# A fused retention, routed-experts and gated-unit kernel on one core: low halves of streamed pieces moved from GpSimd to VectorE, one visit for the one-hot matrix

## The chip, the cores and the metric

The kernel runs on one core of a Trainium2 chip. The metric is the device time of one execution in microseconds (us).

## The reference

Three layers follow one another on N = 3072 tokens of width 512.

```
state = gamma*state + k_t v_t ;  y_t = scale * q_t state        # retention: 4 batches, 8 heads, 768 steps
logits = x @ w_gate                                              # [3072, 8]
order = argsort(-logits.flatten())                               # greedy: best (token, expert) pairs first,
  a token is given once, an expert takes at most cap = 384 tokens
out[mask_e] = relu(x[mask_e] @ w1[e]) @ w2[e]                    # w1 512x1024, w2 1024x512
gate = sigmoid(x @ Wg);  val = x @ Wv                            # Wg, Wv 512x1536
result = (gate * val) @ w_out                                    # 1536x512
```

## The kernel before, in words

**First stage (lines 262 to 638).** Retention over 24 units of 128 tokens. It writes the rows of x to memory and the router's logits to on-chip memory. GpSimd splits the first 16 resident weight pieces there.

**Second stage (lines 640 to 1226).** Eight rounds, one for each expert in the order in which experts fill. Every float32 operand is split into a high half (ScalarE copies it into a fp32r tile) and a low half (raw minus high), and each product is three matmuls: high by high, high by low, low by high (`three`, L1114; L1116 to L1118, and L1194 to L1196 for the output products). A round on TensorE, written out by hand in `one_round` (L1120), is:

- `h_tile(g)`, g = 0..7: 4 steps each, a step being 3 matmuls of 384 columns;
- `h2_tile(m)`, m = 0..3: 8 steps each;
- `gate_val(f)`, f = 0..11: 4 steps for the gate, 4 for the value, and after each but the first `out_products(f-1)`: 3 steps of 3 matmuls of 512 columns;
- four times three transposes of the next expert's gathered rows (L1111), and the last `out_products(11)`.

**Streamed pieces.** Of weights, 24 pieces of 128x512 go through an 8-deep ring in each round: 8 of w1, 8 of w2, 8 of w_out. SP loads one when its slot is free, ScalarE makes its high half (`piece_high`, L760), GpSimd its low half (`piece_low`, L711, an operation of L714), each in the order of the pieces. Only the first eight low halves of round 0 are made by VectorE (`first_low`, L997). Twelve resident pieces come late: ScalarE splits off their high halves before round 0 and GpSimd their low halves in round 0, two behind each streamed piece from number 16 on (`late_low`, L707, an operation of L259). They are first needed in `gate_val(8)`.

**Routing.** While round i runs, VectorE and TensorE find expert i+1 and its 384 tokens together. TensorE makes "visits": small matmuls between two steps, at places fixed by `visit_at` (L101), counted in matmul columns at 2200 to the planned microsecond. TensorE waits at a visit, in order, until VectorE's part (`route(vis)`, L876) is ready. There are 7 digits of 3 visits. The first visit of a digit (L1075) needs the comparison `above` (L852), which VectorE makes from `prefix` (L892) after the digit before. Then come a tie visit, a count visit, a rank visit (V_RANK, number 23, L1097), and four visits (L1102) with 6 one-hot matrices each, held in two buffers of six. After the last one VectorE computes the row numbers and prepares the next routing (`route_ids`, `close`, `prepare`, L960, L952, L856), as one unbroken run of small operations, and GpSimd gathers the rows (`gather`, L699).

**VectorE's order.** `one_round` (L1007) writes it out: before each main operation, `route_until(at)` puts in the routing parts whose planned time has come. The main operations are `h_low(g)`, `h2_low(m)`, and for every f `product(f)` (pf, L991, needs the value part of f) and, after ScalarE's ph (L784), `p_low(f)` (pl, L995), which `out_products(f)` needs. Planned times from the code: `h_end` runs 2.1 to 16.8, `h2_end` 20.9 to 33.5, `val_end[f]` = 37.7, 41.9, 48.2, 54.5, 60.7, 67.0, 73.3, 79.6, 85.9 and so on; `out_end[f-1]` is 2.1 after `val_end[f]`.

```
DIGIT_GAP, LATE_GAP, PART_GAP = us(6.8), us(5), us(4)
while vis[0] < VISITS and (vis[0] == 0 or visit_at[vis[0] - 1 - (vis[0] > V_IDS)] <= at): route(...)
if vis[0] == VISITS and visit_at[VISITS - 1] <= at: route_ids(i + 1); close(); prepare()
```

Of the kernel before, what the change touches and what calls it, by code (L numbers as in the profile page):

```python
# [16 lines left out]
def retention_moe_glu_kernel(nc, q, k, v, w_router, w1, w2, w_gate, w_val, w_out, decay, out):  # L17
# [14 lines left out]
    with ctx:  # L32
# [3 lines left out]
        def sem(name):  # L36
            return ctx.enter_context(nc.semaphore(name))
# [39 lines left out]
        PARTS = U // TPART  # L77
        VISITS = V_IDS + PARTS

# [17 lines left out]
        def us(t):  # L97
            return int(t * COLUMNS_PER_US)

        DIGIT_GAP, LATE_GAP, PART_GAP = us(6.8), us(5), us(4)  # L100
        visit_at = [us(1) + vis // 3 * DIGIT_GAP + us((0, 1.7, 4)[vis % 3]) for vis in range(3 * DIGITS)]  # L101
        visit_at += [visit_at[-1] + (n + 1) * LATE_GAP for n in range(4)]
        visit_at += [visit_at[-1] + (n + 1) * PART_GAP for n in range(PARTS - 1)]
        expert_at = visit_at[V_RANK]
        ids_at = visit_at[-1] + us(2)
        SPLIT_AFTER = us(5)
# [64 lines left out]
        at_above = nc.sbuf_base  # L171
        onehot = sb("onehot", [P, 2, TPART, P], BF16)

# [20 lines left out]
        ring_raw = [placed(f"ring_raw{n}", [P, 512], F32, at_ring + (2 * n + 1) * 512 * 4) for n in range(RING)]  # L194
        above = placed("above", [P, U, RADIX], BF16, at_above)
        digit_i = placed("digit_i", [P, DIGITS, U], I32, at_above)
# [3 lines left out]
        gate = placed("gate", [P, 2, CAP], F32, at_hh + 6 * CAP * 4)  # L200
        xg = placed("xg", [P, TT, DM], F32, at_hl)
        orow = placed("orow", [P, TT, DM], F32, at_h2l)
        shared = at_big + (RESIDENT - 3) * 2 * 512 * 4
# [7 lines left out]
        half_compared = sem("half_compared")  # L211
        route_done = sem("route_done")
        dve_chain = sem("dve_chain")
        expert_known = sem("expert_known")
# [482 lines left out]
        @block.gpsimd  # L697
        def _(pool):
            def gather(i):  # L699

                pool.wait_ge(ids_ready, i + 1)
                pool.sem_inc(ids_seen, 1)
                for j in range(TT):
                    pool.indirect_dma_start(out=xg[:, j, :], out_offset=None, in_=xrows[:, :],
                                            in_offset=bass.IndirectOffsetOnAxis(ap=ids[:, j:j + 1], axis=0)).then_inc(x_gathered, 16)

            def late_low(k):  # L707
                pool.wait_ge(resident_hi, EARLY + k + 1)
                resident_low(EARLY + k)

            def piece_low(i, n):  # L711
                s = n % RING
                pool.wait_ge(piece_hi, STREAMED * i + n + 1)
                nc.gpsimd.tensor_tensor(ring[:, s, 1, :], ring_raw[s][:, :], ring[:, s, 0, :].bitcast(F32),  # L714
                                        ALU.subtract).then_inc(piece_lo, 1)

            def scatter(i):
                pool.wait_ge(ids_kept, i + 1)
                nc.gpsimd.tensor_copy(out_ids[:, :], ids_all[:, bass.ds(i, 1), :].rearrange("p o j -> p (o j)")).then_inc(out_ids_ready, 1)
                pool.wait_ge(out_ids_ready, i + 1)  # L720
                for j in range(TT):
                    pool.wait_ge(orow_ready, TT * (i + 1) + j + 1)
                    pool.sem_inc(orow_seen, 1)
                    pool.indirect_dma_start(out=out[:, :], out_offset=bass.IndirectOffsetOnAxis(ap=out_ids[:, j:j + 1], axis=0),  # L724
                                            in_=orow[:, j, :], in_offset=None).then_inc(scattered, 16)
                pool.wait_ge(scattered, 16 * TT * (i + 1))
                pool.sem_inc(orow_free, 1)

            def one_round(i, follows, late):
                gathered = not follows  # L730
                for n in range(RING, STREAMED + RING if follows else STREAMED):
                    if not gathered and split_at[n] > ids_at:
                        pool.wait_ge(h_done, EVACUATED * (i + 1))
                        gather(i + 1)
                        gathered = True
                    piece_low(i, n)
                    if n >= 2 * RING:
                        for k in late[:2]:
                            late_low(k)
                        late = late[2:]  # L740
                if not gathered:
                    pool.wait_ge(h_done, EVACUATED * (i + 1))
                    gather(i + 1)
                scatter(i)

            gather(0)
            pool.wait_ge(piece_lo, RING)
            one_round(0, True, list(range(LATE)))
            with pool.Fori(1, E - 1) as i:
                one_round(i, True, [])  # L750
            one_round(E - 1, False, [])

# [69 lines left out]
        def _(dve):  # L822
# [53 lines left out]
            def route(vis, i):  # L876
# [3 lines left out]

                dve.wait_ge(route_done, i * VISITS + vis - (vis > V_IDS))
                if vis < V_TIE and vis % 3 == 1:
# [53 lines left out]
                elif vis == V_IDS:  # L936
# [7 lines left out]
                    link(nc.vector.scalar_tensor_tensor(row[:, :], thirds[:, :], -float(P), PS_K[:, 0:U], ALU.mult, ALU.add))  # L944
                if vis >= V_IDS:
                    n = vis - V_IDS
                    for t in range(TPART):
                        tile = n * TPART + t
                        last = nc.vector.tensor_scalar(onehot[:, n % 2, t, :], column[:, :], row[:, tile:tile + 1], None, ALU.is_equal)
                    last.then_inc(route_ready, 1)  # L950

# [44 lines left out]

            def first_low(n):  # L997
                dve.wait_ge(piece_hi, n + 1)
                nc.vector.tensor_tensor(ring[:, n, 1, :], ring_raw[n][:, :], ring[:, n, 0, :].bitcast(F32),
                                        ALU.subtract).then_inc(piece_lo, 1)  # L1000
# [6 lines left out]
            def one_round(i, follows):  # L1007
                vis = [0 if follows else VISITS + 1]

                def route_until(at):  # L1010

                    while vis[0] < VISITS and (vis[0] == 0 or visit_at[vis[0] - 1 - (vis[0] > V_IDS)] <= at):
                        route(vis[0], i + 1)
                        vis[0] += 1
                    if vis[0] == VISITS and visit_at[VISITS - 1] <= at:
                        route_ids(i + 1)
                        close()
                        prepare()
                        vis[0] += 1
# [3 lines left out]
                for g in range(KF):  # L1023
                    route_until(h_end[g] + us(0.3))
                    h_low(i, g)
                for m in range(KD):
                    route_until(h2_end[m] + us(0.3))
                    h2_low(i, m)
                for f in range(KG):
                    route_until(val_end[f])  # L1030
                    product(i, f)
                    route_until(val_end[f] + us(0.4))
                    p_low(i, f)
                assert vis[0] == VISITS + 1
                if follows:
# [11 lines left out]
            for vis in range(VISITS):  # L1047
                route(vis, 0)
            route_ids(0)
            close()  # L1050
            prepare()
            assert link_count[0] == ROUTE_CHAIN, link_count[0]
            for n in range(RING // 2):
                first_low(n)
            for a in range(KD):
                x_low(0, a)
            for n in range(RING // 2, RING):
                first_low(n)
            with dve.Fori(0, E - 1) as i:
# [4 lines left out]
        def _(pe):  # L1064
            pe.wait_ge(tables_made, TABLES)

            def visit(vis, i):
                if vis < V_TIE and vis % 3 == 0:

                    for t in range(0, U, FOLD):  # L1070
                        if t == 0:
                            pe.wait_ge(half_compared, i * DIGITS + vis // 3 + 1)
                        if t == U // 2:
                            pe.wait_ge(route_ready, i * VISITS + vis + 1)
                        last = nc.tensor.matmul(PS_R[:, 0:FOLD * E], above[:, t:t + FOLD, :].rearrange("p t r -> p (t r)"),  # L1075
                                                choice[:, :, t:t + FOLD], start=t == 0, stop=t == U - FOLD)
                    last.then_inc(route_done, 1)
                    return
                pe.wait_ge(route_ready, i * VISITS + vis + 1)
                if vis < V_TIE and vis % 3 == 1:  # L1080
# [18 lines left out]
                else:  # L1099
                    n = vis - V_IDS  # L1100
                    for t in range(TPART):
                        last = nc.tensor.matmul(PS_R[:, 0:2 * TT], onehot[:, n % 2, t, :],  # L1102
                                                slot_ids[:, n * TPART + t, :, :].rearrange("p j n -> p (j n)"),
                                                start=n == 0 and t == 0, stop=n == PARTS - 1 and t == TPART - 1)
                last.then_inc(route_done, 1)
# [156 lines left out]
```

## Time and profile before

| | |
|---|---|
| median of 3 runs | 1146.23 us (1145.22 to 1147.03) |
| the profiled execution | 1147.63 us, its span 1145.9 us |
| TensorE busy with matmuls | 1074.8 us of the span (94%) |
| VectorE busy | 563.3 us (49%) |
| ScalarE busy | 340.0 us (30%) |
| GpSimd busy | 368.0 us (32%) |
| mean granted TensorE clock | 0.971 of 2.4 GHz |

A profile is one execution. "Busy" counts the time in which an engine has an instruction in work. A wait is time in which an engine had none, and is put down to what ended it. Matmuls overlap one another, so that a matmul of 334 ns may be followed by the next after 174 ns.

### The profile page before, as it was taken

The page shows a single profiled execution, that of the slowest core. Times are in us where ns is not written, and L with a number is a line of the kernel's source. Part 1 is how long each engine was busy: PE and PEld are TensorE (multiplying, and loading weights), DVE is VectorE, ACT ScalarE, POOL GpSimd, SP SyncE. Part 2 cuts the span into 40 slices and gives each one's busy share as a digit, 9 for nine tenths or more (in the row PEclk, how much of TensorE's full clock was granted, in tenths as well). Part 3 has the DMA queues.
Part 4 walks back from the last instruction along what each step waited for, and adds up shares of the span by engine and source line. Part 5 has one row for each costly group of instructions (what it writes and reads, how often), then busy time and mean ns, then how long its engine had stood idle before and what let it go on. Part 6 is the DMA issues. An engine that isn't in the chain of part 4 may idle for free.

```text
span 1145.9 us, 20263 instructions
## 1 busy us (share of the span) xinstructions
PE 1074.8 (94%) x7544; PEld 989.7 (86%) x7544; DVE 563.3 (49%) x1431; ACT 340.0 (30%) x635; POOL 368.0 (32%) x357
## 2 busy tenths in 40 slices
PE   5999932989999999999999999999999999999996
PEld 5999922978999889998999899989998999899995
DVE  3555458565445554565356535563456356631111
ACT  2433322322233123412341234222322232224211
POOL 5443401480325042503250416041513151325101
PEclk9999965989999999999999999999999999999998
DMA  9999443311222122312231213121303140304000
GB/s 203 239 225 222 126 129 101 93 56 42 61 83 93 37 65 74 102 38 65 65 111 33 68 56 113 31 69 55 111 23 88 38 126 21 92 19 147 19 1 28
DMA packets 172960, 96.47 MB, mean 84 GB/s; under 512 B 80224, under 2 KB 158048, under 8 KB 172896
## 3 DMA queue, kind: packets, MB, share of 16 engines
q1 hardware_dynamic: 169056, 82.92, 27.1%
q0 software_dynamic: 3840, 12.59, 3.5%
q8 instruction: 53, 0.87, 0.3%
q14 instruction: 11, 0.09, 0.0%
HBM read 82.90 MB, written 12.58 MB: 83 GB/s over the span
## 4 chain that ended last, share of the span: by engine, by line
PE 75%; DVE 8%; issue 2%; POOL 0%; ACT 0%; DMA 0%; DVEq 0%; POOLq 0%
PE bank L1116 19%; PE bank L1118 18%; PE bank L1117 18%; PE bank L1194 6%; PE bank L1195 5%; PE bank L1196 5%; DVE above L852 2%; PE bank L1111 1%; DVE prefix L892 1%; PE bank L1075 1%; PE bank L1083 1%; DVE best L858 0%; DVE top L866 0%; PE bank L1102 0%; ACT ph L784 0%
## 5 line engine op out<-in xcount | busy, mean ns | idle before, releaser
L714 POOL TENSOR_TENSOR ring<-ring_raw,ring 128x512 fp32r<-128x512 f32 x184 | 238.3, 1300 | 435.6 <-ACT ring L764 420.9
L1116 PE MATMUL bank<-h2h,resident 128*128 128x384 f32 x768 | 263.8, 343 | 0.6 <-DVE h2l L982 0.2
L1118 PE MATMUL bank<-h2h,resident 128*128 128x384 f32 x768 | 258.6, 337 | 0.0
L1117 PE MATMUL bank<-h2l,resident 128*128 128x384 f32 x768 | 258.2, 336 | 0.0
L1116 PEld LDWEIGHTS bank<-h2h,resident 128*128 128x128 f32 x768 | 144.8, 189 | 4.5 <-DVE h2l L982 1.1
L1117 PEld LDWEIGHTS bank<-h2l,resident 128*128 128x128 f32 x768 | 144.8, 189 | 3.1
L1118 PEld LDWEIGHTS bank<-h2h,resident 128*128 128x128 f32 x768 | 144.6, 188 | 0.0
L764 ACT ACTIVATE ring<-ring_raw 128x512 fp32r<-128x512 f32 x192 | 117.5, 623 | 64.7 <-DMA ring_raw<-in_moe_w_out_dram 40.7
L991 DVE TENSOR_TENSOR pf<-bank,gate 128x384 f32<-128x384 f32 x96 | 53.1, 553 | 169.9 <-PE bank L1118 166.2
L784 ACT ACTIVATE ph<-pf 128x384 fp32r<-128x384 f32 x96 | 50.4, 525 | 245.5 <-DVE pf L991 245.5
L780 ACT ACTIVATE gate<-bank 128x384 f32<-128x384 f32 x96 | 47.1, 491 | 214.2 <-PE bank L1118 214.2
L1116 PE MATMUL bank<-xh,ring 128*128 128x384 f32 x256 | 90.9, 355 | 0.0
L1116 PE MATMUL bank<-hh,ring 128*128 128x384 f32 x256 | 90.6, 354 | 0.0
L1118 PE MATMUL bank<-xh,ring 128*128 128x384 f32 x256 | 86.5, 338 | 0.0
L1117 PE MATMUL bank<-xl,ring 128*128 128x384 f32 x256 | 86.4, 337 | 0.0
L1118 PE MATMUL bank<-hh,ring 128*128 128x384 f32 x256 | 85.9, 336 | 0.0
L1117 PE MATMUL bank<-hl,ring 128*128 128x384 f32 x256 | 85.8, 335 | 0.0
L724 POOL DMA_INDIRECT out_dram<-orow,out_ids x24 | 23.7, 986 | 183.0 <-DVE orow L1005 178.2
L1194 PE MATMUL bank<-ring,ph 128*128 128x512 f32 x192 | 78.5, 409 | 3.9 <-DVE pl L995 3.9
L995 DVE TENSOR_TENSOR pl<-pf,ph 128x384 fp32r<-128x384 f32 x96 | 54.4, 567 | 52.6 <-ACT ph L784 52.6
L1195 PE MATMUL bank<-ring,ph 128*128 128x512 f32 x192 | 76.2, 397 | 0.0
L1196 PE MATMUL bank<-ring,pl 128*128 128x512 f32 x192 | 76.1, 397 | 0.0
(168 smaller groups left out, 1745.1 us busy)
## 6 DMA issues: line engine op xcount, KB each, us to landing
ring_raw<-in_moe_w_dram SPq DMA_DIRECT2D x128, 256.0 KB, 3.0
ring_raw<-in_moe_w_out_dram SPq DMA_DIRECT2D x64, 256.0 KB, 2.9
qraw<-in_q_dram SPq DMA_DIRECT2D x24, 256.0 KB, 4.0
kraw<-in_k_dram SPq DMA_DIRECT2D x24, 256.0 KB, 4.8
vraw<-in_v_dram SPq DMA_DIRECT2D x24, 256.0 KB, 5.0
xrows<-xrow SPq DMA_DIRECT2D x24, 256.0 KB, 2.9
resident_raw<-in_moe_w_gate_dram SPq DMA_DIRECT2D x12, 256.0 KB, 4.6
resident_raw<-in_moe_w_val_dram SPq DMA_DIRECT2D x12, 256.0 KB, 4.7
```

Source lines behind the costliest of these rows:

```text
L714: nc.gpsimd.tensor_tensor(ring[:, s, 1, :], ring_raw[s][:, :], ring[:, s, 0, :].bitcast(F32), ALU.subtract).then_inc(piece_lo, 1)
L764: nc.scalar.activation(ring[:, n % RING, 0, :], ring_raw[n % RING][:, :], ACT.Copy).then_inc(piece_hi, 1)
L780: nc.scalar.activation(gate[:, f % 2, :], bank[2 * (f % 2)][:, 0:CAP], ACT.Sigmoid).then_inc(gate_ready, 1)
L784: nc.scalar.activation(ph[:, f % 2, :], pf[:, f % 2, :], ACT.Copy).then_inc(ph_ready, 1)
L991: nc.vector.tensor_tensor(pf[:, f % 2, :], bank[2 * (f % 2) + 1][:, 0:CAP], gate[:, f % 2, :], ALU.mult).then_inc(p_ready, 1)
L995: nc.vector.tensor_tensor(pl[:, f % 2, :], pf[:, f % 2, :], ph[:, f % 2, :].bitcast(F32), ALU.subtract).then_inc(pl_ready, 1)
L1116: nc.tensor.matmul(ps, wh, xhi, start=start, stop=False)
L1117: nc.tensor.matmul(ps, wh, xlo, start=False, stop=False)
L1118: return nc.tensor.matmul(ps, wl, xhi, start=False, stop=stop)
L1194: nc.tensor.matmul(PS_OUT[j][:, :], ph[:, f % 2, toks], wh, start=f == 0, stop=False)
L1195: nc.tensor.matmul(PS_OUT[j][:, :], ph[:, f % 2, toks], wl, start=False, stop=False)
L1196: last = nc.tensor.matmul(PS_OUT[j][:, :], pl[:, f % 2, toks], wh, start=False, stop=f == KG - 1)
```

## The change

VectorE makes all the low halves of streamed pieces, put into its written order by `splits_until`. GpSimd no longer makes them; its late resident ones are made one at a time in round 0, each after a gate or a value part of `gate_val(0)` to `gate_val(5)`. The 24 one-hot matrices get a buffer of their own, in the half of `hl` that the gathered rows leave free; VectorE makes them in four parts right behind one another without waiting for TensorE, and TensorE uses them in one visit. `above` no longer shares the one-hot buffers' memory.

```diff
-        VISITS = V_IDS + PARTS
+        VISITS = V_IDS + 1
-        DIGIT_GAP, LATE_GAP, PART_GAP = us(6.8), us(5), us(4)
+        DIGIT_GAP, LATE_GAP, PART_GAP = us(6.8), us(5), us(2)
-        visit_at += [visit_at[-1] + (n + 1) * LATE_GAP for n in range(4)]
-        visit_at += [visit_at[-1] + (n + 1) * PART_GAP for n in range(PARTS - 1)]
+        visit_at += [visit_at[-1] + (n + 1) * LATE_GAP for n in range(3)]
         expert_at = visit_at[V_RANK]
+        part_at = [expert_at + us(1) + n * PART_GAP for n in range(PARTS)]
+        visit_at += [part_at[-1] + LATE_GAP]
         ids_at = visit_at[-1] + us(2)
-        onehot = sb("onehot", [P, 2, TPART, P], BF16)
+        above = sb("above", [P, U, RADIX], BF16)
-        above = placed("above", [P, U, RADIX], BF16, at_above)
+        onehot = placed("onehot", [P, U, P], BF16, at_hl + TT * DM * 4)
...
 # gpsimd
-            def one_round(i, follows, late):
-                gathered = not follows
-                for n in range(RING, STREAMED + RING if follows else STREAMED):
-                    if not gathered and split_at[n] > ids_at:
-                        pool.wait_ge(h_done, EVACUATED * (i + 1))
-                        gather(i + 1)
-                        gathered = True
-                    piece_low(i, n)
-                    if n >= 2 * RING:
-                        for k in late[:2]:
-                            late_low(k)
-                        late = late[2:]
-                if not gathered:
+            def one_round(i, follows):
+                if follows:
                     pool.wait_ge(h_done, EVACUATED * (i + 1))
                     gather(i + 1)
                 scatter(i)
             gather(0)
-            pool.wait_ge(piece_lo, RING)
-            one_round(0, True, list(range(LATE)))
+            for k in range(LATE):
+                pool.wait_ge(val_done if k % 2 else gate_done, k // 2 + 1)
+                late_low(k)
...
 # vector
-                if vis >= V_IDS:
-                    n = vis - V_IDS
-                    for t in range(TPART):
-                        tile = n * TPART + t
-                        last = nc.vector.tensor_scalar(onehot[:, n % 2, t, :], column[:, :], row[:, tile:tile + 1], None, ALU.is_equal)
-                    last.then_inc(route_ready, 1)
+            def make_onehot(n, i):
+                if n == 0 and not (isinstance(i, int) and i == 0):
+                    dve.wait_ge(h_done, EVACUATED * i)
+                for tile in range(n * TPART, (n + 1) * TPART):
+                    last = nc.vector.tensor_scalar(onehot[:, tile, :], column[:, :], row[:, tile:tile + 1], None, ALU.is_equal)
+                last.then_inc(onehot_ready, 1)
-            def first_low(n):
+            def piece_low(i, n):
...
+                def splits_until(at):
+                    while split[0] < (STREAMED + RING if follows else STREAMED) and split_at[split[0]] + us(1.2) <= at:
+                        piece_low(i, split[0])
+                        split[0] += 1
                 def route_until(at):
-                    while vis[0] < VISITS and (vis[0] == 0 or visit_at[vis[0] - 1 - (vis[0] > V_IDS)] <= at):
+                    while vis[0] < VISITS and (vis[0] == 0 or visit_at[vis[0] - 1] <= at):
                         route(vis[0], i + 1)
                         vis[0] += 1
+                    while vis[0] == VISITS and part[0] < PARTS and part_at[part[0]] <= at:
+                        make_onehot(part[0], i + 1)
+                        part[0] += 1
...
                     h_low(i, g)
+                    splits_until(h_end[g])
...
                     h2_low(i, m)
+                    splits_until(h2_end[m])
...
                     p_low(i, f)
+                    splits_until(val_end[f] + us(2))
...
 # tensor
-                    n = vis - V_IDS
-                    for t in range(TPART):
-                        last = nc.tensor.matmul(PS_R[:, 0:2 * TT], onehot[:, n % 2, t, :], ...
+                    for t in range(U):
+                        if t % TPART == 0:
+                            pe.wait_ge(onehot_ready, i * PARTS + t // TPART + 1)
+                        last = nc.tensor.matmul(PS_R[:, 0:2 * TT], onehot[:, t, :], ...
```

## Rows read from the trace of the kernel before

**Rows 1.** The page's first part: busy time and share of the span, by engine.

```profile
PE 1074.8 (94%) x7544; PEld 989.7 (86%) x7544; DVE 563.3 (49%) x1431; ACT 340.0 (30%) x635; POOL 368.0 (32%) x357
```

**Rows 2.** Waits from 200 us on: engine, line, waited for; total us, times, longest.

```profile
PE bank L1075 <- DVE above L852: 5.3, 5, 1.3
PE bank L1194 <- DVE pl L995: 3.9, 7, 0.6
```

**Rows 3.** The chain that ended last: transposes that open rounds 0, 1 and 2; start, length.

```profile
196.97 2.82 PE bank L1111 x12
...
323.64 1.31 PE bank L1111 x12
...
440.40 1.31 PE bank L1111 x12
```

**Rows 4.** Stretches of round 0: length, busy by engine, granted clock, DMA share, GB/s.

```profile
230.00:240.00 10.00, 8.70 (x59) 8.11 (x58) 6.56 (x9) 3.13 (x6) 10.00 (x8) 1.00 0.28 100
240.00:250.00 10.00, 8.16 (x44) 7.18 (x44) 5.13 (x8) 3.60 (x7) 10.00 (x9) 0.83 0.18 54
250.00:260.00 10.00, 7.57 (x41) 6.25 (x40) 6.05 (x9) 0.91 (x2) 4.13 (x3) 0.83 0.00 0
```

**Rows 5.** TensorE in order of time, round 0: start, length, instruction, idle before it.

```profile
233.19 0.24 PE L1075 MATMUL bank<-choice,above 128*128 128x32 bf16 x3 [1.30 <-DVE above L852]
...
242.53 0.24 PE L1075 MATMUL bank<-choice,above 128*128 128x32 bf16 x3 [1.30 <-DVE above L852]
...
253.07 0.24 PE L1075 MATMUL bank<-choice,above 128*128 128x32 bf16 x3 [1.13 <-DVE above L852]
254.61 0.26 PE L1075 MATMUL bank<-choice,above 128*128 128x32 bf16 x3 [1.29 <-DVE above L852]
```

**Rows 6.** VectorE (round 0, then round 1) and GpSimd (round 0) in order of time.

```profile
238.00 1.31 DVE L892 SCALAR_TENSOR_TENSOR prefix<-prefix,bank,digit_f 128x24 f32<-128x24 f32 x1 [1.85 <-PE bank L1087]
239.35 3.13 DVE L852 TENSOR_TENSOR above<-prefix,ladder 128x384 bf16<-128x384 f32 x2
...
332.79 0.25 DVE L892 SCALAR_TENSOR_TENSOR prefix<-digit_f,bank 128x24 f32<-128x24 f32 x1
333.07 1.02 DVE L852 TENSOR_TENSOR above<-prefix,ladder 128x384 bf16<-128x384 f32 x2
...
240.48 3.13 POOL L259 TENSOR_TENSOR resident<-resident_raw,resident 128x512 fp32r<-128x512 f32 x2
```

**Rows 7.** Groups by line: low halves on GpSimd, then those on VectorE (ns: least, median, most).

```profile
L714 POOL TENSOR_TENSOR ring<-ring_raw,ring 128x512 fp32r<-128x512 f32 x184 | 238.3, 1300 | 435.6 <-ACT ring L764 420.9
...
L999 DVE TENSOR_TENSOR ring<-ring_raw,ring x8: 681/682/683, 195.3 to 202.6; 128x512 fp32r<-128x512 f32 x8
```

**Rows 8.** The last visit of round 1 and what follows it, TensorE and VectorE.

```profile
410.45 0.31 PE L1102 MATMUL bank<-slot_ids,onehot 128*128 128x6 bf16 x6
...
410.80 0.16 DVE L963 TENSOR_REDUCE id_sums<-bank 128x3 f32<-128x6 f32 x1 [3.21 <-PE bank L1102]
...
417.44 0.55 DVE L991 TENSOR_TENSOR pf<-bank,gate 128x384 f32<-128x384 f32 x1
418.58 0.56 DVE L995 TENSOR_TENSOR pl<-pf,ph 128x384 fp32r<-128x384 f32 x1 [0.59 <-ACT ph L784]
...
419.29 0.47 PE L1194 MATMUL bank<-ring,ph 128*128 128x512 f32 x1 [0.57 <-DVE pl L995]
```

**Rows 9.** Two steps of `gate_val` on TensorE, first matmul of each.

```profile
416.48 0.33 PE L1116 MATMUL bank<-h2h,resident 128*128 128x384 f32 x1
...
417.00 0.33 PE L1116 MATMUL bank<-h2h,resident 128*128 128x384 f32 x1
```

**Rows 10.** Round 1 around digit visit 18: VectorE, then TensorE.

```profile
369.51 0.56 DVE L995 TENSOR_TENSOR pl<-pf,ph 128x384 fp32r<-128x384 f32 x1 [0.59 <-ACT ph L784]
369.99 0.24 DVE L892 SCALAR_TENSOR_TENSOR prefix<-prefix,bank,digit_f 128x24 f32<-128x24 f32 x1
...
372.47 0.32 PE L1075 MATMUL bank<-choice,above 128*128 128x32 bf16 x6
```

More of the change, by code:

```diff
@@ L201, in retention_moe_glu_kernel @@
         xg = placed("xg", [P, TT, DM], F32, at_hl)
+        onehot = placed("onehot", [P, U, P], BF16, at_hl + TT * DM * 4)
+        assert TT * DM * 4 + U * P * 2 <= KF * CAP * 4
         orow = placed("orow", [P, TT, DM], F32, at_h2l)
@@ L212, in retention_moe_glu_kernel @@
         route_done = sem("route_done")
+        onehot_ready = sem("onehot_ready")
         dve_chain = sem("dve_chain")
@@ L709, in late_low @@
                 resident_low(EARLY + k)
[L711 to L715, printed above, removed]
             def scatter(i):
@@ L746, in _ @@
             gather(0)
-            pool.wait_ge(piece_lo, RING)
-            one_round(0, True, list(range(LATE)))
-            with pool.Fori(1, E - 1) as i:
-                one_round(i, True, [])
-            one_round(E - 1, False, [])
+            for k in range(LATE):
+                pool.wait_ge(val_done if k % 2 else gate_done, k // 2 + 1)
+                late_low(k)
+            with pool.Fori(0, E - 1) as i:
+                one_round(i, True)
+            one_round(E - 1, False)
         @block.scalar
@@ L879, in route @@
                     return
-                dve.wait_ge(route_done, i * VISITS + vis - (vis > V_IDS))
+                dve.wait_ge(route_done, i * VISITS + vis)
                 if vis < V_TIE and vis % 3 == 1:
@@ L995, in p_low @@
                 nc.vector.tensor_tensor(pl[:, f % 2, :], pf[:, f % 2, :], ph[:, f % 2, :].bitcast(F32), ALU.subtract).then_inc(pl_ready, 1)
-            def first_low(n):
-                dve.wait_ge(piece_hi, n + 1)
-                nc.vector.tensor_tensor(ring[:, n, 1, :], ring_raw[n][:, :], ring[:, n, 0, :].bitcast(F32),
+            def piece_low(i, n):
+                s = n % RING
+                dve.wait_ge(piece_hi, STREAMED * i + n + 1)
+                nc.vector.tensor_tensor(ring[:, s, 1, :], ring_raw[s][:, :], ring[:, s, 0, :].bitcast(F32),
                                         ALU.subtract).then_inc(piece_lo, 1)
@@ L1008, in one_round @@
                 vis = [0 if follows else VISITS + 1]
+                part = [0]
+                split = [RING]
+                def splits_until(at):
+                    while split[0] < (STREAMED + RING if follows else STREAMED) and split_at[split[0]] + us(1.2) <= at:
+                        piece_low(i, split[0])
+                        split[0] += 1
                 def route_until(at):
-                    while vis[0] < VISITS and (vis[0] == 0 or visit_at[vis[0] - 1 - (vis[0] > V_IDS)] <= at):
+                    while vis[0] < VISITS and (vis[0] == 0 or visit_at[vis[0] - 1] <= at):
                         route(vis[0], i + 1)
                         vis[0] += 1
+                    while vis[0] == VISITS and part[0] < PARTS and part_at[part[0]] <= at:
+                        make_onehot(part[0], i + 1)
+                        part[0] += 1
                     if vis[0] == VISITS and visit_at[VISITS - 1] <= at:
@@ L1033, in one_round @@
                     p_low(i, f)
+                    splits_until(val_end[f] + us(2))
+                splits_until(out_end[-1])
                 assert vis[0] == VISITS + 1
@@ L1048, in _ @@
                 route(vis, 0)
+            for n in range(PARTS):
+                make_onehot(n, 0)
             route_ids(0)
@@ L1053, in _ @@
             for n in range(RING // 2):
-                first_low(n)
+                piece_low(0, n)
             for a in range(KD):
@@ L1057, in _ @@
             for n in range(RING // 2, RING):
-                first_low(n)
+                piece_low(0, n)
             with dve.Fori(0, E - 1) as i:
@@ L1073, in visit @@
                         if t == U // 2:
-                            pe.wait_ge(route_ready, i * VISITS + vis + 1)
+                            pe.wait_ge(route_ready, i * (VISITS - 1) + vis + 1)
                         last = nc.tensor.matmul(PS_R[:, 0:FOLD * E], above[:, t:t + FOLD, :].rearrange("p t r -> p (t r)"),
@@ L1078, in visit @@
                     return
-                pe.wait_ge(route_ready, i * VISITS + vis + 1)
+                if vis < V_IDS:
+                    pe.wait_ge(route_ready, i * (VISITS - 1) + vis + 1)
                 if vis < V_TIE and vis % 3 == 1:
@@ L1099, in visit @@
                 else:
-                    n = vis - V_IDS
-                    for t in range(TPART):
-                        last = nc.tensor.matmul(PS_R[:, 0:2 * TT], onehot[:, n % 2, t, :],
-                                                slot_ids[:, n * TPART + t, :, :].rearrange("p j n -> p (j n)"),
-                                                start=n == 0 and t == 0, stop=n == PARTS - 1 and t == TPART - 1)
+                    for t in range(U):
+                        if t % TPART == 0:
+                            pe.wait_ge(onehot_ready, i * PARTS + t // TPART + 1)
+                        last = nc.tensor.matmul(PS_R[:, 0:2 * TT], onehot[:, t, :], slot_ids[:, t, :, :].rearrange("p j n -> p (j n)"),
+                                                start=t == 0, stop=t == U - 1)
                 last.then_inc(route_done, 1)
```

## The prediction, made before the changed kernel was built or run

> **What bounds the kernel now.** I read the page's busy times first: TensorE has a matmul in work for 1074.8 of 1145.9 us, VectorE for 563.3, GpSimd for 368.0 [rows 1]. So only time in which TensorE stands or is clocked down can be won. The chain that ended last shows the length of a round by the transposes that open it: 440.40 - 323.64 = 116.76 us for round 1, but 323.64 - 196.97 = 126.67 us for round 0 [rows 3]. The other rounds repeat round 1. The waits from 200 us on say what is lost: 5.3 us for `above`, all in round 0, and 3.9 us for `pl`, once in each of the seven rounds in which a routing runs [rows 2]. The stretches of round 0 add that the granted clock averaged 0.83 in two spans of 10 us [rows 4]. In round 0 GpSimd is busy for all of 230 to 250 us [rows 4], and just there VectorE's `prefix` and `above` take 1.31 and 3.13 us instead of 0.25 and 1.02 [rows 6]. TensorE waits for them, 1.30 us at 233.19, 1.30 at 242.53, 1.13 and 1.29 around 253 to 255 [rows 5]. The rest of the span (retention, the first routing, the last scatter) holds the same instructions in the same order after the change, but for the one-hot parts of the first routing, where VectorE's rate sets the pace in both. I count it at zero.
>
> **Round 0, what is won.** The twelve late low halves no longer run in a block with the streamed ones. Won: the 5.3 us of waits, and the clock. Two spans of 10 us at 0.83 lose 1.7 us each, 3.4 together, less about 0.3 for standing inside the second. Sum 8.4. The cross-check is round 0 against round 1: 9.9 longer, though it lacks the `out_products(11)` of a round before (2.1 planned), while its cold start costs about 3 (1.5 in the transposes, 2.82 against 1.31 [rows 3], and as much again in the matmuls behind them). That leaves 9.9 + 2.1 - 3 = 9.0. I take 8.8.
>
> **Round 0, what comes in its place.** The late halves now start when a gate or value part ends. Number 1 meets `pl(0)`, number 2 meets the comparison for digit visit 18, with the new piece operations 21 and 22 in between. At worst each of the two holds VectorE for one whole GpSimd operation, 1.3 [rows 7], 2.6 together. At best nothing. The row of `above` at 239.35, 3.13 us beside two GpSimd operations of 3.13 us [rows 6], is nearest to the bad end, but there the operations came without a gap, and here with gaps of 2 us and more. I take 1.5. The Trainium skill's page SBUF — State Buffer, section Who interferes with whom, has a VectorE instruction with two inputs in SBUF and a GpSimd one that reads SBUF exclude each other for a whole instruction. The long `above` agrees; by the rule alone this term would stand at its upper end and the total 1.1 higher.
>
> **Low halves on VectorE.** 184 operations of 0.682 us [rows 7] are 125 us, 15.7 of work to a round; with 563.3 busy of 1145.9 [rows 1] there is room, so what counts is where they stand. `splits_until` puts numbers 8 to 23 behind `hl3` to `hl7`, `h2l0` to `h2l3`, `pl0` and `pl1`, and 24, 25 behind `pl5`; 26, 27 behind `pl6`; one each behind `pl7` to `pl10`. ScalarE's high half is earlier in every case, and TensorE needs none of them within 5 us. The cover fails in one place: 21 and 22 stand between `pl0` and the comparison for visit 18. In round 1 `pl0` starts at 369.51 and `prefix` at 369.99 [rows 10]. With 1.36 more, `prefix` starts at 371.4, and 1.27 later `above` is whole, 372.7; the visit comes at 372.47 and needs its second half about 0.1 later. Wait about 0.2 to 0.3, and 0 to 0.6 as bounds, as GpSimd's own collisions with `prefix` and `above` are gone. Take 0.3 a round. TensorE's small standing before `gate_val(0)` (its `h2l` behind a late `above`) goes: -0.1. For removing GpSimd's streamed work nothing else is won, since all of it was hidden in rounds 1 to 7.
>
> **Four visits in one.** A visit of six takes 0.31 us on the trace [rows 8], and about 0.25 of TensorE's time. One of 24 keeps the matmuls and saves three entries: 0 to 0.4, take 0.24 a round.
>
> **The visit moves, and this is the costly part.** Planned times: rank visit at 60.8. Before: visits at 65.8, 69.8, 73.8, 77.8. After: parts made at 61.8 to 67.8, one visit at 67.8 + 5 = 72.8. TensorE stops only after a step. Before, 77.8 is passed three steps ahead of `val_end[7]` = 79.6. After, 72.8 is passed only with the last step of the value part of `gate_val(6)` (the step before ends at 72.79). VectorE's `route_until(val_end[6])` sees 72.8 <= 73.3, and so puts `route_ids`, `close` and `prepare` ahead of `product(6)`, as it did before ahead of `product(7)`. VectorE arrives early and waits there, with `pf`, `ph` and `pl` of f = 6 behind it, and GpSimd's gather behind the row numbers. The run is one chain: from the visit at 410.45 + 0.31 to `id_sums` at 410.80, `pf` 417.44, `pl` 418.58, first output matmul 419.29 [rows 8], 8.5 us in which nothing can be left out. TensorE had, before, three value steps, `out_products(6)` and `gate_val(8)` to do meanwhile, and still stood 0.57 [rows 8]. After, it has `out_products(5)` and `gate_val(7)`, the same without three steps. A step is 417.00 - 416.48 = 0.52 us [rows 9], so the stand grows by 1.57 to some 2.1 us. It falls in every one of the seven rounds with a routing. Bounds: 1.2, if GpSimd's absence makes the chain shorter (no GpSimd arithmetic ran beside it, so little), and 1.9 if it lengthens it.
>
> Per round: 1.57 + 0.3 - 0.1 - 0.24 = 1.53; times seven, 10.7.
>
> **The clock.** In round 0 the 1.30 us wait at 233.19 was followed by no fall: 1.00 up to 240 us. The interrupted stand that ends at 243 and the one of 1.13 and 1.29 us with three small matmuls between were each followed by a stretch at 1.2 GHz [rows 4, 5], 1.7 us each. The new stand, 2.1 us in one, lies between those and nearer to the latter. I estimate a fall in five of the seven rounds, at 1.6: 8.0. Bounds 0 and 7 x 1.7 = 12.
>
> **Sum.** -8.8 + 1.5 + 10.7 + 8.0 = +11.4. The profiled execution (1147.63 us, span 1145.9 and 1.7 around it) lies 1.4 above the median 1146.23, so 1159.0 by it and 1157.6 by the median. I forecast **1157.5**; own range 1152 to 1163. A measurement of this kernel can tell about 0.2%, 2.3 us, from no change.
>
> **Rivals.**
> - **The stand comes, the clock holds.** Speaks for it: a 1.30 us wait cost no clock, and the stand stays short of the two that did. Against: only by a few tenths. Price: the 8.0 goes, 1149.5, range 1147 to 1152. The Trainium skill's page TensorE: Matmul & The Clock Gate, section Why this matters for your kernels, warns only of idle gaps longer than this one; by that rule this rival wins, while the two falls of round 0, where small matmuls broke the gaps, speak against it. Chance 0.30.
> - **Faster: the closing chain does not hold TensorE longer.** Its place is between the visit and `out_products(6)`. If the chain took 1.57 us less than the 8.5 of [rows 8], the waits stay as they are: -8.8 + 1.5 + 7 x (-0.04) = -7.6, 1138.6. It decides at a chain under about 7.0 us; between 7.0 and 8.2 the two parts cancel. For it: VectorE operations get shorter without GpSimd elsewhere [rows 6]. Against: the chain ran beside none of GpSimd's arithmetic. Chance 0.10, and 0.05 for a result within 0.2% by such a part cancellation.
> - **VectorE becomes late in the digits.** If each of the seven digits costs TensorE 0.3 instead of one, 7 x 6 x 0.3 = 12.6 more, some 1168. Only visit 18 has a piece operation straight before its comparison, which speaks against. Chance 0.08.
> - **The change does not do what it says**, for instance if the compiler's order kept the late halves together: then only 8.8 is lacking, 1166. Chance 0.02.
>
> **Numbers.** The forecast keeps 0.45. Slower by over 0.2% (above 1148.5) is 0.45 + 0.08 + 0.02 and three quarters of the clock rival, 0.22: 0.77. Within: 0.05 and the rest of that rival, 0.13. Faster: 0.10. The range leaves out the faster cases and the far ones: 1147 to 1163.
>
> **What would show it.** In the profile after: rounds 1 to 6 near 118.3 us plus 1.7 where the clock fell, round 0 near 121 to 123; the waits of L1194 for `pl` 15 us in seven times, none over 2.3, at f = 6; the waits of L1075 after 200 us under 4 us, on visit 18; clock 0.5 for some 3 us behind each stand; `prefix` at 0.25 us throughout rounds 1 to 6. It is wrong if the waits for `pl` stay near 0.6, or if rounds 1 to 6 are not longer than 116.8.

## The result and the profile after

The changed kernel takes 1157.43 us (median of 4 runs, 1153.2 to 1158.2) against 1146.63 us for the kernel before on the same chip. The ratio is 1.0094, 95% interval 1.0071 to 1.0116: slower by 10.8 us. The profiled execution took 1157.16 us, its span 1155.4.

The page of the changed kernel, its busy times and the granted clock in 40 slices; they answer to [rows 1].

```profile
PE 1076.7 (93%) x7544; PEld 993.9 (86%) x7544; DVE 612.3 (53%) x1615; ACT 340.2 (29%) x635; POOL 130.0 (11%) x173
...
PEclk9999965999999999999999999999999999999998
```

TensorE's instructions are the same in number. VectorE has 184 more and 49 us more work, GpSimd 238 us less. VectorE's busy time grew by less than the 126 us of the streamed halves, because its other operations got shorter. Over rounds 1 to 6 `prefix`, `above` and the one-hot operations, the same in number, took 22.0, 51.5 and 45.6 us before, and 7.4, 37.0 and 24.5 after. So GpSimd's halves did cost VectorE some 8 us in every round; the last experiment shows that TensorE waited for none of it there. The slices of the clock are too coarse to show what follows.

TensorE's waits from 200 us on in the changed kernel: engine, line, waited for; total us, times, longest. They answer to [rows 2].

```profile
PE bank L1200 <- DVE pl L983: 14.7, 7, 2.2
PE bank L1080 <- DVE above L839: 1.8, 2, 1.3
PE bank L1089 <- DVE partial L871: 0.2, 1, 0.2
```

The wait for `above` fell from 5.3 to 1.8 us, the one for `pl` rose from 3.9 to 14.7.

The chain that ended last, transposes that open rounds 0, 1, 2, 3 and 7 of the changed kernel (start, length), answers to [rows 3].

```profile
196.11 2.84 PE bank L1117 x12
...
317.29 1.31 PE bank L1117 x12
...
436.56 1.31 PE bank L1117 x12
...
555.86 1.31 PE bank L1117 x12
...
1033.45 1.31 PE bank L1117 x12
```

Round 0 takes 121.18 us instead of 126.67. Round 1 takes 119.27 instead of 116.76, and rounds 1 to 6 together 716.16. Before they took 700.55 (from 323.64 to 1024.19). The span's books close: the start 0.86 earlier, round 0 5.49 shorter, rounds 1 to 6 15.61 longer, the last round and its scatter 0.24 longer, together +9.5 = 1155.4 - 1145.9. The medians lie 10.8 apart: the profiled execution of the kernel before was 1.0 above its median (1147.63 against 1146.63), that of the changed kernel 0.3 below.

The end of the routing in round 1 of the changed kernel, TensorE and VectorE in order of time. It answers to [rows 8].

```profile
398.49 0.76 PE L1109 MATMUL bank<-slot_ids,onehot 128*128 128x6 bf16 x24
...
399.29 0.16 DVE L951 TENSOR_REDUCE id_sums<-bank 128x3 f32<-128x6 f32 x1 [2.98 <-PE bank L1109]
...
405.84 0.55 DVE L979 TENSOR_TENSOR pf<-bank,gate 128x384 f32<-128x384 f32 x1
406.98 0.56 DVE L983 TENSOR_TENSOR pl<-pf,ph 128x384 fp32r<-128x384 f32 x1 [0.59 <-ACT ph L771]
...
407.68 0.76 PE L1200 MATMUL bank<-ring,ph 128*128 128x512 f32 x1 [2.09 <-DVE pl L983]
```

A stand is time in which TensorE has no matmul in work. VectorE waited for the visit from 396.3 on, with `product(6)` behind the wait. From `id_sums` to `pf` it takes 6.55 us, before 6.64: the chain is the same. TensorE stood 2.09 us until `pl` was made.

The granted clock behind that stand, in stretches of the changed kernel (length, busy by engine with counts, clock, DMA share, GB/s):

```profile
407.00:408.00 1.00, 0.32 (x1) 0.35 (x2) 1.00 (x2) 0.84 (x2) 0.00 (x0) 0.76 0.00 0
408.00:409.00 1.00, 1.00 (x3) 0.81 (x3) 1.00 (x3) 0.00 (x0) 0.00 (x0) 0.50 0.00 0
409.00:410.00 1.00, 1.00 (x4) 0.71 (x4) 0.41 (x2) 0.76 (x2) 0.00 (x0) 0.50 0.06 16
410.00:411.00 1.00, 1.00 (x4) 0.81 (x3) 0.96 (x2) 0.28 (x1) 0.00 (x0) 0.53 0.00 0
411.00:412.00 1.00, 1.00 (x7) 0.90 (x6) 0.00 (x0) 0.00 (x0) 0.00 (x0) 1.00 0.00 0
```

Half clock, 1.2 GHz, for over 3 us. One minus the clock, summed, is 1.71 us. The same is seen behind the stand in each of rounds 1 to 6, not in round 0, and once in round 0 behind the waits for `above`: seven falls, 11.9 us of clock, against two and 3.4 before. One of the four timed runs, at 1153.2 us, had a mean clock of 0.971 where the others had 0.965 and 0.966. At 1.71 us to a fall, 0.005 of 1155 us are some three falls fewer, an estimate, as that run has no trace.

### The profile page after: what moved, and what is told of

Read it like the earlier page. It is cut to its first block, busy times and chain, and to the rows that moved or that the text cites. A ratio compares the mean times of both kernels' runs of the same rounds, so it can differ in the third digit from the quotient of the medians.

```text
span 1155.4 us, 20307 instructions
## 1 busy us (share of the span) xinstructions
PE 1076.7 (93%) x7544; PEld 993.9 (86%) x7544; DVE 612.3 (53%) x1615; ACT 340.2 (29%) x635; POOL 130.0 (11%) x173
## 4 chain that ended last, share of the span: by engine, by line
PE 76%; DVE 7%; issue 2%; ACT 0%; POOL 0%; DMA 0%; DVEq 0%; POOLq 0%
PE bank L1122 19%; PE bank L1124 18%; PE bank L1123 18%; PE bank L1200 6%; PE bank L1201 6%; PE bank L1202 6%; DVE above L839 1%; PE bank L1117 1%; PE bank L1080 1%; PE bank L1089 1%; DVE best L845 0%; DVE top L853 0%; PE bank L1109 0%; ACT ph L771 0%; DVE onehot L937 0%
## 5 line engine op out<-in xcount | busy, mean ns | idle before, releaser
L988 DVE TENSOR_TENSOR ring<-ring_raw,ring 128x512 fp32r<-128x512 f32 x192 | 126.2, 683 | 0.0
L1200 PE MATMUL bank<-ring,ph 128*128 128x512 f32 x192 | 82.2, 428 | 14.7 <-DVE pl L983 14.7
L707 POOL DMA_INDIRECT xg<-xrows,ids x24 | 23.8, 990 | 519.9 <-DVE ids L953 515.1
L1201 PE MATMUL bank<-ring,ph 128*128 128x512 f32 x192 | 80.3, 418 | 0.0
L1202 PE MATMUL bank<-ring,pl 128*128 128x512 f32 x192 | 79.6, 415 | 0.0
```

The lines of the kernel that those rows point to most:

```text
L988: nc.vector.tensor_tensor(ring[:, s, 1, :], ring_raw[s][:, :], ring[:, s, 0, :].bitcast(F32), ALU.subtract).then_inc(piece_lo, 1)
L1200: nc.tensor.matmul(PS_OUT[j][:, :], ph[:, f % 2, toks], wh, start=f == 0, stop=False)
L1201: nc.tensor.matmul(PS_OUT[j][:, :], ph[:, f % 2, toks], wl, start=False, stop=False)
L1202: last = nc.tensor.matmul(PS_OUT[j][:, :], pl[:, f % 2, toks], wh, start=False, stop=f == KG - 1)
```

## The experiments

**The visit put back.** One number of the changed kernel.

```diff
-        visit_at += [part_at[-1] + LATE_GAP]
+        visit_at += [part_at[-1] + us(10)]
```

> The changed kernel with its one visit put at 77.8 instead of 72.8 planned us, so that the closing chain again stands ahead of product(7) and TensorE again has three value steps more to do beside it; the low halves stay on VectorE. Theory (the place of the visit makes the stand, the stand makes the clock fall): the waits for pl go from 14.7 back to about 4 us in seven times, no fall of the clock in rounds 1 to 6, so 1157.4 - 7 x 1.5 - 6 x 1.7 = about 1137. Rival (the low halves on VectorE make the rounds longer): rounds stay near 119.3, total 1155 or more.

Measured: 1137.47 us, ratio to the kernel before 0.9932 (0.9915 to 0.9948). The waits for `pl` are 3.2 us in seven times, round 2 (433.00 to 549.14) takes 116.14 us, and the clock falls once, in round 0. That is 20 us below the changed kernel, or 19 when each is counted against the kernel before on its own chip. So much hangs on where its one visit stands, and without them the change is a gain. The low halves on VectorE do not lengthen a round.

**One step earlier.** Again one number, and TensorE gets one step of 0.52 us [rows 9] more beside the chain.

```diff
-        visit_at += [part_at[-1] + LATE_GAP]
+        visit_at += [part_at[-1] + us(4.9)]
```

> The changed kernel with its one visit one step of gate_val earlier (72.7 planned us, passed at 72.79). The stand for pl must shrink by one step, 0.52, to about 1.57 us in each of seven rounds, -3.6 in all. What it tells apart is the clock: if a stand of 1.6 us is still followed by a fall as those of 2.1 were, about 1153.8; if it is not, as after the 1.30 us wait of the kernel before, about 1143.6.

Measured: 1144.48 us, ratio 0.9995 (0.9986 to 1.0005). TensorE's waits from 200 us on:

```profile
PE bank L1200 <- DVE pl L983: 11.2, 7, 1.6
```

The stand of round 1, TensorE in order of time, and the clock over it (a stretch, columns as above):

```profile
407.72 0.47 PE L1200 MATMUL bank<-ring,ph 128*128 128x512 f32 x1 [1.64 <-DVE pl L983]
```

```profile
406.00:411.00 5.00, 3.36 (x17) 2.92 (x17) 3.82 (x7) 2.47 (x5) 0.00 (x0) 1.00 0.06 21
```

The stands, now 1.5 to 1.65 us, shrank by 3.5 us in all and the time by 13 (11 by the ratios to the kernel before). None of the seven was followed by a fall. The rest, some 8 to 9.5, is the clock. By rounds, round 2 takes 117.37 us (435.10 to 552.47) against 119.30 (436.56 to 555.86), of which 0.52 is the step. Over rounds 2 to 6 the difference is 2.07 a round. So a fall costs 1.4 to 1.6 us of time, a little less than the 1.71 of clock. In five of the six rounds the slow stretch starts only when the stand is over. But its 512-column matmuls start 0.43 us apart (408.67, 409.10, 409.52) against 0.23 at full clock, less than double.

**Only the place of the visits, on the kernel before.** GpSimd keeps the low halves, and there are four visits.

```diff
-        DIGIT_GAP, LATE_GAP, PART_GAP = us(6.8), us(5), us(4)
+        DIGIT_GAP, LATE_GAP, PART_GAP = us(6.8), us(5), us(7 / 3)
```

> The kernel before with nothing changed but the gap of the four one-hot visits, 2.33 instead of 4 planned us, so that the last comes at 72.8 as in the changed kernel. GpSimd keeps the low halves. Theory: the stand for pl grows to 2.1 us in seven rounds (+11) and the clock falls behind about six of them (+10): about 1167. Rival (it takes the single visit or the low halves on VectorE): 1146 to 1148.

Measured: 1165.05 us, ratio 1.0169 (1.0152 to 1.0186). TensorE's waits from 200 us on:

```profile
PE bank L1194 <- DVE pl L995: 14.0, 7, 2.0
PE bank L1075 <- DVE above L852: 5.4, 5, 1.3
```

The clock falls behind six of the seven stands. The one round without a fall, round 3, has the same stand, 1.99 us, and takes 118.31 us (566.17 to 684.48) where rounds 1, 2, 4, 5 and 6 take 119.7 to 119.9: the price of a fall once more, 1.4 to 1.6 us, with nothing else changed. This one number alone costs 20 us (1165.05 against 1144.89 on that chip), so it takes neither the single visit nor the low halves on VectorE.

**The chain taken out of the way.** In the changed kernel only `route_ids` stays ahead of `product(6)`.

```diff
                         route_ids(i + 1)
-                        close()
-                        prepare()
+                        closing[0] = True
                         vis[0] += 1
...
                     p_low(i, f)
+                    if closing[0]:
+                        close()
+                        prepare()
+                        closing[0] = False
                     splits_until(val_end[f] + us(2))
```

> The changed kernel with close and prepare behind p_low(6) instead of ahead of product(6); only the row numbers stay ahead. If the chain ahead of product(6) is the whole cause, no wait for pl is left (0 of 14.7 us), no fall of the clock in rounds 1 to 6, rounds of about 116: 1157.4 - 14.7 - 10.2 = about 1132.5. If VectorE is too full for the chain anywhere, a wait of about the same size comes up one or two f later and the time stays above 1145.

Measured: 1132.07 us, ratio 0.9887 (0.9871 to 0.9904). There is no wait for `pl` at all, and rounds take 115.5 us (661.82 to 777.37). What is left from 200 us on is the wait for `above` in round 0 and 0.2 us for `partial`:

```profile
PE bank L1084 <- DVE above L839: 1.8, 2, 1.3
PE bank L1093 <- DVE partial L871: 0.2, 1, 0.2
```

VectorE has room for the chain where nothing hangs on it.

**The same on the kernel before**, with `close` and `prepare` behind `p_low(7)`, where the chain then stands; the edit is the one above, without `splits_until`.

> The kernel before with close and prepare behind p_low(7) instead of ahead of product(7), nothing else. The wait for pl of 0.57 us in seven rounds goes, and nothing comes instead: 1146.6 - 7 x 0.6 = about 1142. Rival: the chain then makes product(8) late and a wait comes up for pl(8): 1146.

Measured: 1139.73 us, ratio 0.9937 (0.9919 to 0.9956); rounds of 115.95 us (436.44 to 552.39) instead of 116.76. So the wait shown as 0.57 cost 0.8 us a round. Most of the difference is how idle time is counted: from the end of a matmul of 334 ns, while in a dense row the next starts after 174. In its profile the clock fell once where it had fallen twice. Beside the 115.5 of the run before this one, one visit instead of four is worth about 0.45 us a round. The last experiment bears it out: with the single visit and GpSimd making the streamed halves, as here, rounds 1 to 6 take 115.5.

**The late halves singly, on the kernel before.** One behind each streamed half instead of two; GpSimd still makes both.

```diff
-                        for k in late[:2]:
+                        for k in late[:1]:
                             late_low(k)
-                        late = late[2:]
+                        late = late[1:]
```

> The kernel before with one late resident low half behind each streamed one instead of two; the streamed ones stay on GpSimd. If the gain of round 0 comes from breaking up GpSimd's unbroken run, the waits for above after 200 us fall from 5.3 to 2 us or less, round 0 has no fall of the clock, and the time is about 1146.6 - 7 = 1139.6. If it takes VectorE making the streamed ones, at most 2 us are won: 1144.6 or more.

Measured: 1141.37 us, ratio 0.9967 (0.9951 to 0.9983). TensorE's waits from 200 us on:

```profile
PE bank L1194 <- DVE pl L995: 4.6, 7, 1.2
PE bank L1075 <- DVE above L852: 2.8, 4, 1.3
```

No fall of the clock in round 0, which takes 121.51 us (196.10 to 317.61) instead of 126.67. Breaking up GpSimd's run is worth 5.2 us of round 0 in the profile and 3.7 by the medians, of the 8.8 that I put down to the change in round 0. It is less than I expected of it: half of the waits stay, and the stand for `pl` in round 0 grew to 1.2.

**The late halves away from the digits, on the changed kernel.**

```diff
-            for k in range(LATE):
-                pool.wait_ge(val_done if k % 2 else gate_done, k // 2 + 1)
+            for k in range(8):
+                pool.wait_ge(val_done if k % 2 else gate_done, k // 2 + 3)
                 late_low(k)
-            with pool.Fori(0, E - 1) as i:
+            pool.wait_ge(h_done, EVACUATED)
+            gather(1)
+            pool.wait_ge(gate_done, 9)
+            for k in range(8, LATE):
+                late_low(k)
+            scatter(0)
+            with pool.Fori(1, E - 1) as i:
```

> The changed kernel with the late resident low halves moved away from the digits in round 0: eight behind the gate and value parts of f = 2 to 5, four in a row from gate part 8 on. The waits for above at visit 18 of round 0 (0.54 and 1.29 us) and the fall of the clock behind them (1.7) go: 1157.4 - 3.5 = about 1154. If they collide elsewhere instead: 1157.

Measured: 1154.7 us, ratio 1.0078 (1.005 to 1.0106). The waits for `above` are gone, and so is the fall behind them; round 0 takes 117.65 us (196.18 to 313.83), 3.5 less. The medians show 2.7 less, the ratios to the kernel before 1.8, so 3.5 is the profile's price for the collision at visit 18 in the changed kernel, whose rows are below. The next run gives 3.9 for the same step.

**Both together.**

> The changed kernel with close and prepare behind p_low(6), and with the late resident low halves away from the digits. The two gains add, as they lie in different places: about 1132.5 - 3.5 = 1129. All waits of TensorE after 200 us under 1 us, mean clock 0.977.

Measured: 1128.14 us, ratio 0.9846 (0.9821 to 0.9871), and again, on another occasion:

> The fastest version again, on the same chip as the run with GpSimd's streamed low halves, for the comparison of the two: 1128.1 us, 1.5% below the kernel before.

1128.56 us, ratio 0.9857 (0.9841 to 0.9873). It beats both kernels. In the profile of the first of the two TensorE waits for nothing between 200 us and the last scatter, in that of the second 0.2 us for `partial`. The mean clock is 0.975 and 0.974 in these profiles, not 0.977.

**And with the streamed halves given back to GpSimd.** The kernel of the last two runs, with VectorE's `splits_until` made empty, `piece_low` for numbers from 8 on back on GpSimd as in the kernel before, and the late halves singly behind them.

> The fastest version so far (1128.1 us: single visit, close and prepare behind p_low(6), late halves away from the digits) with the streamed low halves given back to GpSimd and one late resident half behind each from number 16 on. It prices what moving the streamed halves to VectorE is worth when nothing else is in the way. Theory (they were hidden on GpSimd in rounds 1 to 7, so the move earns only in round 0): rounds 1 to 6 stay at 115.5, round 0 keeps about 3 us of waits for above as in the run with the late halves singly: about 1131.5. Rival (GpSimd's operations cost every round something through VectorE): 0.5 us or more in each of eight rounds besides, 1135 or more.

Measured: 1136.7 us, 0.9935 (0.9918 to 0.9951), 8.1 slower than the kernel it was compared with. The theory holds for rounds 1 to 6: 115.44, 115.47 and 115.61 us for the first three, as with the halves on VectorE. The time lies above the 1135 that I had given to the rival, but not for the rival's reason. The theory missed round 0: 122.31 us (196.23 to 318.54) against 115.31 (197.74 to 313.05). One wait there I had not foreseen; TensorE, VectorE and GpSimd in order of time:

```profile
284.74 0.30 PE L1124 MATMUL bank<-slot_ids,onehot 128*128 128x6 bf16 x6 [2.73 <-DVE onehot L950]
...
277.22 7.46 DVE L950 TENSOR_SCALAR onehot<-column,row 128x128 bf16<-128x128 bf16 x6
...
278.41 1.29 POOL L262 TENSOR_TENSOR resident<-resident_raw,resident 128x512 fp32r<-128x512 f32 x1
279.67 1.29 POOL L717 TENSOR_TENSOR ring<-ring_raw,ring 128x512 fp32r<-128x512 f32 x1
280.91 1.28 POOL L262 TENSOR_TENSOR resident<-resident_raw,resident 128x512 fp32r<-128x512 f32 x1
```

Six one-hot operations take 7.46 us beside six GpSimd operations without a gap; with GpSimd idle six take 1.06. About one gets in behind each GpSimd operation. In rounds 1 and 2 the same six still take 4.28 us each time, and TensorE does not wait: that cost is real and hidden.

So the streamed halves on VectorE are worth nothing to TensorE in the steady rounds. The 7 us of round 0 belong to the pair: this run also puts the late halves back between the streamed ones. What the streamed halves on GpSimd would cost with the late ones still away from the digits was not tried. The other 1.1 of the 8.1 is not placed. The two profiles lie only 5.5 us apart, because the one with the halves on VectorE has a fall of the clock more in the first stage and starts round 0 1.5 us later.

The wait of 2.73 us is the longest stand of all these runs behind 200 us, and no fall follows it. Stretches over it, columns as above:

```profile
282.00:284.00 2.00, 0.00 (x1) 0.00 (x0) 2.00 (x3) 0.00 (x0) 2.00 (x3) 1.00 0.00 0
284.00:285.00 1.00, 0.27 (x7) 0.27 (x8) 0.68 (x1) 0.00 (x0) 0.63 (x1) 1.00 0.00 0
285.00:287.00 2.00, 2.00 (x11) 1.67 (x10) 1.07 (x5) 0.65 (x2) 0.00 (x0) 1.00 0.04 8
```

## Why the prediction was right

The forecast was 1157.5 us, +11.4 on the median; the median moved by 10.8. Step by step:

- **The visit moves.** Right in cause and size. I had 1.57 us more in each of seven rounds, to some 2.1. Measured: 2.0 to 2.2, at f = 6. Shown by moving nothing but the visits in either kernel: minus 19 to 20 us in the changed one, plus 20 in the one before.
- **The clock.** Right in kind, a little low. I had five falls at 1.6; behind the stand there were six of seven in the profile, at about 1.5 us of time. The rival in which the clock holds is refuted for this kernel's stands of 2.1 us. It is what happens at 1.6. The Trainium skill's page TensorE: Matmul & The Clock Gate, section Why this matters for your kernels, warns only of idle gaps longer than all of these and would have let the clock hold in both. The traces do not agree: stands of 2.0 to 2.2 were followed by a fall in 18 of 21 cases over three profiled kernels, stands of 1.5 to 1.65 in none of 7. But I ordered the cases by the length of the stand ("between those and nearer to the latter"), and length alone does not decide: the 2.73 us above brought no fall, nor did the 2.02 us in round 0 of the changed kernel. What else it takes stays open.
- **Round 0, what is won.** The waits and both falls went, but I had costed them low. With the late halves away from the digits round 0 is 9.0 shorter than before, although its stand is 1.57 longer and its one visit saves 0.45: 10.1 won where I had 8.8. The same comes out of the fastest kernel, whose round 0 is 11.4 shorter with no stand at all. Counting the waits without the overlap of matmuls explains 0.8 of the missing 1.3 (an estimate: five waits at 0.334 - 0.174 = 0.16); the rest is open. And the cause was drawn too wide: the run with the late halves singly wins 5.2 in round 0 with GpSimd still making all the halves.
- **Round 0, what comes in its place.** I took 1.5 us of waits at visit 18 and measured 0.54 + 1.29. I left out the fall of the clock behind them, 1.7. VectorE, then GpSimd, then TensorE in round 0 of the changed kernel:

```profile
242.14 1.28 DVE L988 TENSOR_TENSOR ring<-ring_raw,ring 128x512 fp32r<-128x512 f32 x2
243.35 1.26 DVE L879 SCALAR_TENSOR_TENSOR prefix<-prefix,bank,digit_f 128x24 f32<-128x24 f32 x1
244.65 2.09 DVE L839 TENSOR_TENSOR above<-prefix,ladder 128x384 bf16<-128x384 f32 x2
...
242.72 1.85 POOL L262 TENSOR_TENSOR resident<-resident_raw,resident 128x512 fp32r<-128x512 f32 x1 [0.92 <-PE bank L1124]
244.81 1.52 POOL L262 TENSOR_TENSOR resident<-resident_raw,resident 128x512 fp32r<-128x512 f32 x1 [0.23 <-PE bank L1124]
...
245.26 0.24 PE L1080 MATMUL bank<-choice,above 128*128 128x32 bf16 x3 [0.54 <-DVE above L839]
246.80 0.24 PE L1080 MATMUL bank<-choice,above 128*128 128x32 bf16 x3 [1.29 <-DVE above L839]
```

`prefix` takes 1.26 us and the two `above` 2.09 where GpSimd's third and fourth late halves lie, numbers 2 and 3 counted from 0. I had foreseen number 2 there and number 1 against `pl(0)`. But `pl(0)`, at 241.62, took 0.60 instead of 0.56 us, and it was number 3 that held up `above`. So the two collisions came as counted, but both at visit 18. GpSimd's own are held up too, 1.85 and 1.52 instead of 1.29.

- **Low halves on VectorE.** The term of 0.3 us a round was mis-sized: it measured zero in rounds 1 to 6. The -0.1 a round, taken for a stand ahead of `gate_val(0)`, had nothing behind it either: in the kernel before TensorE's matmuls wait for `h2l` once, 0.2 us in round 0; later only a weight load does, 0.16 us in four rounds, beside running matmuls. From round 1 of the changed kernel, VectorE, then TensorE:

```profile
363.50 1.28 DVE L988 TENSOR_TENSOR ring<-ring_raw,ring 128x512 fp32r<-128x512 f32 x2
364.71 0.24 DVE L879 SCALAR_TENSOR_TENSOR prefix<-prefix,bank,digit_f 128x24 f32<-128x24 f32 x1
364.98 1.03 DVE L839 TENSOR_TENSOR above<-prefix,ladder 128x384 bf16<-128x384 f32 x2
...
365.98 0.33 PE L1080 MATMUL bank<-choice,above 128*128 128x32 bf16 x6
```

Two piece operations in a row take 1.21 us from start to start of what follows, not 2 x 0.68. `above` is whole at 366.01, and the visit, which needs its second half last, came at 365.98 without a wait. It was a matter of a tenth.
- **Four visits in one.** Mis-sized too: taken at 0.24 us a round, worth about 0.45.
- **The rounds.** I said 118.3 plus 1.7, so about 120, and 121 to 123 for round 0. Measured 119.27 and 121.18. With the measured sizes the sum closes: 116.76 + 1.57 - 0.45 + 1.5 = 119.4, where rounds 1 to 6 took 119.36 on average.

In sums: rounds 1 to 6 were forecast at 6 x 1.53 + 8.0 = 17.2 and came to 15.6, round 0 at -8.8 + 1.5 + 1.53 = -5.8 and came to -5.5. Within each, errors offset one another: a fall too few against 0.5 too much a round, and in round 0 a missed fall against a gain costed low. That the total came within 0.1 us of the median is luck; the place and the size of the stand are not. One rival's total was also added wrongly, 1157.5 + 12.6 being 1170 and not 1168; nothing rested on it.

## What to carry to other kernels

Where the order on an in-order engine is written against planned times, moving an event costs or earns what the consumer still has to do beside the chain behind it. Count the steps between the event and the operation that waits; here three of 0.52 us set the sign of the whole change. Put a long chain that nobody waits for behind, not ahead of, the short operation that the bound engine waits for: it took 5 us from the kernel before and 24 to 25 from the changed one.

## What the hardware showed that I had not expected

- Where these stands of TensorE were 2.0 to 2.2 us long, 18 of 21 were followed by half clock and cost nearly twice their length; at 1.5 to 1.65 us none of 7 was. The step in the time is about 1.5 us a round. It is no rule for every stand: one of 2.73 us passed at full clock.
- Six small VectorE operations starve beside an unbroken run of GpSimd (7.46 us for 1.06): each takes about as long as one GpSimd operation, 1.24 us, instead of 0.18.
- VectorE's loop grew by 24 operations, and with that the packets of the instruction queue rose from 11 to 40 or 41 in every kernel with the halves on VectorE, and stayed at 11 in every one without. The page's rows of the kernel before and of the changed one:

```profile
q14 instruction: 11, 0.09, 0.0%
```

```profile
q14 instruction: 40, 0.33, 0.1%
```

At the start of each of rounds 1 to 6 VectorE stands 1.8 to 2.1 us for nothing that the profile shows, in the kernels with 40 or 41 packets and in none of the others (the kernel after, ahead of the first `partial` of round 1):

```profile
323.75 0.19 DVE L871 CAST partial<-bank 128x32 f16<-128x32 f32 x1 [1.83 <-issue]
```

It is hidden but for 0.2 us at most, once in an execution. That it is the fetching of the longer loop's instructions was not tried.
